# Front of a fused attention, expert and mixing kernel: second buffers for raw queries and keys, one block sum on VectorE, smaller constant load

## Chip, cores, metric

One Trainium2 chip, one core of it. The metric is device time in microseconds (us) for one execution; the time before is the median of 3 runs, 707.57 us (707.03 to 708.71).

## What is computed

Three stages in one launch, all in float32 at the interface. Only the first is touched by the change; the others follow it.

```python
# attention, B=2, H=8, S=768, D=64; nb = 24 blocks of 32 positions
k_sum = k.reshape(B, H, nb, block, D).max(axis=3)
v_sum = v.reshape(B, H, nb, block, D).mean(axis=3)
scores_l = scale * q @ k.T                  # kept where |i - j| < 16, else -1e9
scores_s = scale * q @ k_sum.T + log(block)
a = softmax(concat([scores_l, scores_s]))
x = a @ concat([v, v_sum])                  # (B, S, 512)
# experts: 8, one per token; argmax of x @ w_gate, held over from the token
# before where sigmoid(x @ w_local) >= 0.5; p[e] * (relu(x @ w1[e]) @ w2[e])
# mixing: u = x + real(fft(fft(x, seq), feature)); layer norm;
# out = u + relu(un @ w_ch1) @ w_ch2
```

## The kernel before, in words

Everything is written by hand for the five instruction streams: PE (matmul and transposes), VectorE, ScalarE, POOL (GpSimd) and SP, which only issues transfers. Each stream is in program order and waits on semaphores; the order of the work is the order of the code.

The attention stage goes over 8 **pairs** of heads (`PAIRS`) and in each over 6 **tiles** of 128 queries (`ST`). Pairs 0 to 5 run in a loop of three steps, two pairs in each (`par` is 0 or 1), pairs 6 and 7 behind it.

Raw queries and keys of a pair come in as `q_raw` and `k_raw` (one buffer each before), 192 KB per head and tensor (`load_qk`, L338). PE transposes them in three pieces (`stage`, L1205, the transposes on L1207) into a PSUM bank, ScalarE copies each piece out into `kT` and `qT` (L576, L580, L583). POOL lays `kT` out as windows (`k_win`, L464 to L469); VectorE takes the maxima over blocks of 32 keys (`block_max`, L793), and POOL copies them beside the windows (L476, L477). Pieces for pair i+1 are transposed in tiles 0 to 2 of pair i.

A tile goes: PE scores for both heads (L1234, 184 columns: 160 local and 24 block scores), VectorE adds the mask and takes the row maximum (`mask_scores`, L804), ScalarE the exponential with the row sums (L603), PE transposes the probabilities (L1243), VectorE copies them to SBUF (`probs_out`, L813), PE multiplies with the values (L1254 to L1256), VectorE normalises (L834). Sums are guarded and inverted for two tiles at once (L821, L827). Masks run two tiles ahead. The mask lies in the constants `cst` once for each head of a pair, since the second head has its 184 columns in another order.

The block means of the values: SP loads them with 32 positions of a block side by side (`load_blocks`, L358), 8 KB for each of 24 partitions and head, into `blocks`. The first pair's are summed by one VectorE instruction (L909), all others by POOL in five halving additions (`block_sums`, L489 and L493). The second pair's sum (`block_sums(1, 1, True)`) stands behind POOL's first key windows. ScalarE writes the means into the value tiles (`block_mean_rows`, L592) at the end of tile 5 of the pair before; for the first pair VectorE does it (L915). Both signal `vmean_ok`, which the pair's first value product waits for.

SP issues in this order: identity, keys, queries, the other constants, first blocks, first values (eight transfers, `load_v`, L345), second blocks, three tables of the gate; then, for each pair, keys and queries of the next pair as soon as PE has transposed this one's, blocks of the pair after next, values of the next pair.

In front, VectorE clears `qT`, `probs`, two columns of `x_all` and the edges of `kT` (L782, L783), signals `cleared`, and sends twelve increments to semaphores (L787). POOL clears `blocks`, `vA`, `vB` and `zero_row` (L453 to L456).

After attention come the gate (L1268 transposes, L1276 products; its first product waits for `tables_in`), the routing, the experts and the mixing.

## Time and profile before

| | |
|---|---|
| median of 3 runs | 707.57 us |
| the profiled execution, its own time | 704.34 us |
| its span, first to last instruction | 702.5 us |
| attention stage, by the timeline | about 0 to 110 us |
| PE busy over the span | 617.6 us (88%) |
| VectorE (DVE) busy | 359.5 us (51%) |
| ScalarE (ACT) busy | 259.5 us (37%) |
| POOL busy | 108.6 us (15%) |

Busy times are sums over one engine and overlap with the others. A row of a timeline gives the start in us from the span's start, the duration of the group, engine, source line and operation, what is written and read, how many instructions were merged (x4), and in brackets how long the engine was idle before and what released it. A windows row gives for one stretch the busy us (and instruction count) of PE, PE's weight loads, DVE, ACT and POOL, then the granted clock of TensorE, the busy share of the transfer engines and GB/s. In the names `arena`, `mid` and `small` are large SBUF tensors that hold many tiles (keys, queries, values and probabilities in `arena`, blocks and the row of zeros in `mid`), `bank` is PSUM, and `SPq` is SP's queue.

### The profile page before, as it was taken

To read this page: it belongs to the slowest core of one execution; us is meant where nothing else is said; L and a number is where in the kernel's file an instruction comes from. 1 tells how busy PE (TensorE), PEld (TensorE's weight loads), DVE (VectorE), ACT (ScalarE), POOL (GpSimd) and SP (SyncE) were. 2 spreads that over 40 slices of the span, in tenths; PEclk is the share of its full clock that TensorE was granted. 3 is DMA by queue.
4 is the path that set the end of the run, shared out by engine and by line. 5 is a ranking of instruction groups with operands and counts; after the bars stand their busy time and mean duration, and the time that the engine had idled before them with its cause. 6 is when DMAs were issued, how large, how long until landed. Compare 5 with 4: busy or idle time off the path is not lost.

```text
span 702.5 us, 11006 instructions
## 1 busy us (share of the span) xinstructions
PE 617.6 (88%) x3254; PEld 525.5 (75%) x3255; DVE 359.5 (51%) x893; ACT 259.5 (37%) x576; POOL 108.6 (15%) x132
## 2 busy tenths in 40 slices
PE   4799999411799899999889989999999999999994
PEld 3799999301578678878664468899899899989993
DVE  5788874743424252553326298444544454454442
ACT  3588874102313231441101133444344434434430
POOL 5657540033000010100100002002000040000001
PEclk9999999755889999999999999999999999999998
DMA  7766645046812381124141431000100010000001
GB/s 170 164 140 154 144 141 204 0 146 235 311 43 61 119 276 30 30 60 149 45 156 39 179 121 61 1 1 0 46 1 1 0 45 0 0 33 12 0 0 45
DMA packets 58874, 59.07 MB, mean 84 GB/s; under 512 B 43552, under 2 KB 43680, under 8 KB 57824
## 3 DMA queue, kind: packets, MB, share of 16 engines
q1 hardware_dynamic: 53056, 41.62, 19.7%
q0 software_dynamic: 3776, 13.44, 4.9%
q10 hardware_dynamic: 2016, 3.70, 2.4%
q8 instruction: 13, 0.21, 0.1%
q14 instruction: 13, 0.11, 0.1%
HBM read 43.73 MB, written 15.01 MB: 84 GB/s over the span
## 4 chain that ended last, share of the span: by engine, by line
PE 68%; DVE 9%; issue 8%; ACT 5%; DMA 5%; POOL 2%; SPq 2%; DVEq 1%; ACTq 0%; POOLq 0%
PE bank L1480 18%; PE bank L1467 18%; PE bank L1385 9%; PE bank L1357 7%; PE bank L1234 3%; ACT arena L603 3%; DMA mid<-sorted_x 2%; DVE parts L967 2%; PE bank L1243 2%; POOL sorted_x L516 1%; PE bank L1410 1%; PE bank L1276 1%; PE bank L1423 1%; PE bank L1345 1%; PE bank L1254 1%
## 5 line engine op out<-in xcount | busy, mean ns | idle before, releaser
L967 DVE TENSOR_TENSOR parts<-arena,parts 128x512 fp32r<-128x512 f32 (+1 forms) x152 | 111.5, 773 | 99.3 <-ACT parts L729 78.9
L1467 PE MATMUL bank<-parts 128*128 128x384 f32 x768 | 147.8, 341 | 2.8 <-DVE parts L967 2.8
L1480 PE MATMUL bank<-parts 128*128 128x512 f32 x576 | 143.7, 394 | 0.2
L1467 PEld LDWEIGHTS bank<-parts 128*128 128x128 f32 x768 | 136.8, 190 | 8.6 <-DVE parts L967 4.5
L1480 PEld LDWEIGHTS bank<-parts 128*128 128x128 f32 x576 | 106.8, 188 | 20.9 <-DVE mid L1130 1.1
L1385 PE MATMUL bank<-parts 128*128 128x512 f32 x312 | 77.1, 404 | 5.9 <-DVE parts L967 5.3
L1357 PE MATMUL bank<-parts 128*128 128x512 f32 x312 | 76.3, 401 | 2.1 <-DVE parts L967 2.1
L1385 PEld LDWEIGHTS bank<-parts 128*128 128x128 f32 x312 | 59.5, 194 | 20.0 <-issue 4.7
L729 ACT ACTIVATE parts<-arena 128x512 fp32r<-128x512 f32 x64 | 40.4, 631 | 83.5 <-PE bank L1480 83.5
L1357 PEld LDWEIGHTS bank<-parts 128*128 128x128 f32 x312 | 59.1, 193 | 14.6 <-issue 2.8
L967 DVE TENSOR_TENSOR parts<-bank,parts 128x512 fp32r<-128x512 f32 (+1 forms) x56 | 35.1, 649 | 42.4 <-ACT parts L719 19.7
L753 ACT ACTIVATE parts<-bank 128x384 fp32r<-128x384 f32 x64 | 31.5, 491 | 56.7 <-PE bank L1467 56.7
L1168 DVE SCALAR_TENSOR_TENSOR parts<-bank,parts 128x384 fp32r<-128x384 f32 x64 | 35.6, 557 | 30.9 <-ACT parts L753 30.9
L603 ACT ACTIVATE arena<-arena,small 128x184 f32<-128x184 f32 x96 | 42.1, 440 | 10.3 <-DVE small L804 9.3
L1234 PE MATMUL bank<-arena 128*128 128x184 f32 x192 | 41.1, 340 | 1.3 <-ACT arena L583 1.3
L523 POOL DMA_INDIRECT folded_y<-mid,dest_i x13 | 12.5, 958 | 180.0 <-DVE dest_i L1025 180.0
L724 ACT ACTIVATE parts<-arena 128x512 fp32r<-128x512 f32 x64 | 39.5, 618 | 0.0
L1345 PE MATMUL bank<-cst,mid 128*128 128x128 f32 x56 | 10.0, 308 | 31.9 <-DMA mid<-sorted_x 31.8
L551 POOL DMA_INDIRECT out<-mid,rows_i x6 | 6.1, 1020 | 205.0 <-DVE mid L1130 204.4
L1024 DVE TENSOR_SCALAR mid<-bank,small 128x512 f32<-128x512 f32 x13 | 9.8, 751 | 52.5 <-PE bank L1385 52.5
L489 POOL TENSOR_TENSOR mid<-mid 128x1024 f32<-128x1024 f32 (+3 forms) x28 | 33.7, 1202 | 12.9 <-DMA mid<-in_v 9.2
L1234 PEld LDWEIGHTS bank<-arena 128*128 128x128 f32 x192 | 31.6, 202 | 3.1 <-ACT arena L583 1.7
(174 smaller groups left out, 732.1 us busy)
## 6 DMA issues: line engine op xcount, KB each, us to landing
arena<-in_moe_w SPq DMA_DIRECT2D x24, 512.0 KB, 5.0
sorted_x<-mid POOLq DMA_DIRECT2D x1, 5160.0 KB, 18.3
arena<-in_moe_w_ch SPq DMA_DIRECT2D x2, 2048.0 KB, 8.3
arena<-in_moe_w_ch SPq DMA_DIRECT2D x4, 1024.0 KB, 8.9
mid<-sorted_x ACTq DMA_DIRECT2D x14, 258.0 KB, 3.2
arena<-in_k SPq DMA_DIRECT2D x16, 192.0 KB, 2.7
arena<-in_q SPq DMA_DIRECT2D x16, 192.0 KB, 3.2
mid<-in_v SPq DMA_DIRECT2D x16, 192.0 KB
```

Source lines behind the costliest of these rows:

```text
L489: pool.tensor_tensor(blocks[:, par, 0:n], blocks[:, par, 0:n], blocks[:, par, n:2 * n], ALU.add).then_inc(halved, 1)
L603: last = act.activation(probs[:, t % 3, (2 * NSP - NS) * hh:(2 * NSP - NS) * hh + NS], masked[:, t % 3, hh, :], ACT.Exp, scale=-1.0, bias= ...
L724: act.activation(m1_hi[:, f % 2, :].rearrange("p (c n) -> p c n", c=DC), m1_raw[:, :, P * f:P * f + P], ACT.Copy).then_inc(m1h_ok, 1)
L729: act.activation(m2_hi[:, f % 2, :], m2_raw[:, f, :], ACT.Copy).then_inc(m2h_ok, 1)
L753: act.activation(g_hi[:, f % 2, :], bank[2 + f % 2][:, 0:GN], ACT.Relu).then_inc(ghi_ok, 1)
L967: return dve.tensor_tensor(out, whole, upper.bitcast(F32), ALU.subtract)
L1168: dve.scalar_tensor_tensor(g_lo[:, f % 2, :], bank[2 + f % 2][:, 0:GN], 0.0, g_hi[:, f % 2, :].bitcast(F32), ALU.max, ALU.subtract).then_i ...
L1234: last = pe.matmul(S_BANK[t % 3][:, NS * hh:NS * hh + NS], qT[:, par, hh, P * t:P * t + P], k_win[:, par, t, keys], start=True, stop=True)
L1357: last = pe.matmul(bank[1 + half][:, :], x[:, r], w[:, c, f], start=(c == 0 and x is xT_hi and w is w1_hi), stop=(c == DC - 1 and w is w1_lo))
L1385: last = pe.matmul(bank[5][:, :], x[:, c, :], w[:, c // 2, f], start=(c == 0 and x is hT_hi and w is w2_hi), stop=(c == FC - 1 and w is w2 ...
L1467: last = pe.matmul(bank[2 + f % 2][:, 0:GN], w[:, f % 2, r], x[:, par, c, :], start=(c == 0 and w is m1_hi and x is cT_hi), stop=(c == DC ...
L1480: last = pe.matmul(bank[4 + t][:, :], x[:, f % 2, r], w[:, f % 2, :], start=(f == 0 and x is g_hi and w is m2_hi), stop=(f == MC - 1 and w ...
```

## The change

`q_raw` and `k_raw` get a second buffer, with a semaphore for each (`k_in`, `q_in` become pairs), and SP loads them one pair further ahead. The second pair's blocks are summed by VectorE in one instruction, inside tile 4 of the first pair (a branch around it in the other loop steps). The mask is loaded for the first head alone, and VectorE copies it into `mask2` in the second head's order. The constants that only the routing needs, and the gate's tables, are loaded behind the last values, the former for 8 partitions. VectorE clears `blocks`, and `probs` after the signal `cleared`; POOL clears `zero_row` first and of `vA` only the rows that no load fills. PE starts with two matmuls of 512 columns on `zero_row`, of which nothing is used. In front SP issues values ahead of blocks.

```diff
-    for name, n in (("ident", P), ("mask", 3 * 2 * NS), ("base", NT), ...
+    for name, n in (("ident", P), ("mask", 3 * NS), ("base", NT), ("forced", NT), ("first", E), ("dest", NT),
+                    ("iota", 1), ("thr", NT), ("tri", E), ("slot", SLOTS + 1), ("ones", 1), ("odd", CW), ("expert", E), ("sum", P)):
...
+        late_consts = cols["iota"][0]
-        q_raw = a(ST * P).rearrange("p (t h d) -> p t h d", t=ST, h=2)
+        q_raw = a(2 * ST * P).rearrange("p (b t h d) -> p b t h d", b=2, t=ST, h=2)
...
@@ SP @@
-            load_qk(0)
-            sp.dma_start(cst[:, P:], consts[:, P:]).then_inc(consts_in, 16)
+            load_qk(0, 0)
+            sp.dma_start(cst[:, P:late_consts], consts[:, P:late_consts]).then_inc(consts_in, 16)
             sp.wait_ge(v_cleared, 2)
+            load_v(0, 0)
             sp.wait_ge(blocks_set, 1)
             load_blocks(0, 0)
-            load_v(0, 0)
+            load_qk(1, 1)
             load_blocks(1, 1)
-            sp.dma_start(wg[:, :, 0:E], ...).then_inc(tables_in, 16)
-            sp.dma_start(wg[:, :, E:E + 1], ...).then_inc(tables_in, 16)
-            sp.dma_start(rows_i[:, :], rows).then_inc(tables_in, 16)
             def next_pair(i, par, more=True):
-                sp.wait_ge(qk_ps, 3 * (i + 1))
-                load_qk(i + 1)
                 if more:
+                    sp.wait_ge(qk_ps, 3 * (i + 1))
+                    load_qk(i + 2, par)
                     sp.wait_ge(vsum_ok, i + 1)
                     load_blocks(i + 2, par)
...
             next_pair(PAIRS - 2, 0, False)
+            sp.dma_start(cst[0:E, late_consts:], consts[0:E, late_consts:]).then_inc(tables_in, 16)
+            sp.dma_start(wg[:, :, 0:E], ...).then_inc(tables_in, 16)
+            sp.dma_start(wg[:, :, E:E + 1], ...).then_inc(tables_in, 16)
+            sp.dma_start(rows_i[:, :], rows).then_inc(tables_in, 16)
@@ POOL @@
-            pool.memset(blocks, 0.0).then_inc(blocks_set, 1)
-            pool.memset(vA, 0.0).then_inc(v_cleared, 1)
+            pool.memset(zero_row, 0.0).then_inc(zero_set, 1)
+            pool.memset(vA[0:PRE, :, 0], 0.0).then_inc(v_cleared, 1)
             pool.memset(vB, 0.0).then_inc(v_cleared, 1)
-            pool.memset(zero_row, 0.0).then_inc(zero_set, 1)
...
-                if first:
-                    pool.wait_ge(vsum_ok, 1)
-                else:
-                    pool.wait_ge(vmean_ok, i - 1)
+                pool.wait_ge(vsum_ok, i)
+                pool.wait_ge(vmean_ok, i - 1)
...
-            block_sums(1, 1, True)
@@ VectorE @@
-            for tile in (qT, probs, xa[:, :, DM + 2:XW], kT[:, 0:PRE]):
-                dve.memset(tile, 0.0)
-            link(dve.memset(kT[:, PRE + S:KTW], 0.0))
+            dve.memset(kT[:, 0:PRE], 0.0)
+            dve.memset(kT[:, PRE + S:KTW], 0.0)
+            link(dve.memset(qT, 0.0))
             dve.sem_inc(cleared, 1)
+            dve.memset(blocks, 0.0).then_inc(blocks_set, 1)
+            dve.memset(xa[:, :, DM + 2:XW], 0.0)
+            dve.memset(probs, 0.0).then_inc(rest_cleared, 1)
+            dve.wait_ge(rest_cleared, 1)
             for signal, n in ((att_out, TWO), (masked_ok, THREE), ...
                 dve.sem_inc(signal, n)
...
-  ... in1=mask[:, var_, hh, :],
+  ... in1=(mask, mask2)[hh][:, var_, :],
...
+            def add_blocks(par):
+                dve.tensor_reduce(block_sum[:, par], blocks[:, par].rearrange("p (j d) -> p d j", d=D), axis=AX.X, op=ALU.add).then_inc(vsum_ok, 1)
...
                     if t == 2 and not last_pair:
                         block_max(i + 1, 1 - par)
+                    if t == 4 and par == 0 and not last_pair and not isinstance(i, int):
+                        with dve.If(i < 1):
+                            dve.wait_ge(blocks_in[1], 32)
+                            add_blocks(1)
                 normalise(i, par, ST - 1, out_at(ST - 1))
             block_max(0, 0)
             dve.wait_ge(consts_in, 16)
+            for to, n, at in ((0, NB, WK), (NB, WK - P, P), (NS - P, P, 0)):
+                last = dve.tensor_copy(mask2[:, :, to:to + n], mask[:, :, at:at + n])
+            link(last)
...
             for b in range(B):
                 choose(b)
+            dve.wait_ge(tables_in, 64)
@@ PE @@
+            def keep_warm(columns, times):
+                for _ in range(times):
+                    pe.matmul(bank[0][:, 0:columns], zero_row[:, 0:P], zero_row[:, 0:columns], start=True, stop=True)
+            pe.wait_ge(zero_set, 1)
+            keep_warm(512, 2)
             pe.wait_ge(ident_in, 16)
...
-                    pe.wait_ge(k_in, 32 * (i + 1))
+                    pe.wait_ge(k_in[par], 32 * ((i + 2) // 2))
...
-                    pe.wait_ge(tables_in, 48)
+                    pe.wait_ge(tables_in, 64)
```

How the order of instructions changes at three places. VectorE in front, before:

```order
L782 MEMSET arena 128x3072
L782 MEMSET arena 128x1152
L782 MEMSET x_all 128x12x2
L782 MEMSET arena 128x15
L783 MEMSET arena 128x17
L793 TENSOR_REDUCE arena<-arena 128x24
L904 COPY x_all<-cst 128x12
```

and after the change:

```order
L781 MEMSET arena 128x15
L782 MEMSET arena 128x17
L783 MEMSET arena 128x3072
L785 MEMSET mid 128x4096
L786 MEMSET x_all 128x12x2
L787 MEMSET arena 128x1152
L797 TENSOR_REDUCE arena<-arena 128x24
L914 COPY mask<-cst 128x3x24
L914 COPY mask<-cst 128x3x32
L914 COPY mask<-cst 128x3x128
L918 COPY x_all<-cst 128x12
```

`mid 128x4096` is `blocks`, `arena 128x3072` is `qT`, `arena 128x1152` is `probs`. Clearing of `blocks` and three mask copies have come in, the clearing of `kT` has moved to the front.

SP in front, from the load of the constants on, before:

```order
L361 DMA cst<-consts 128x1712
L358 DMA mid<-in_v 24x2048 x2
L347 DMA arena<-in_v 113x64
L349 DMA arena<-in_v 128x5x64
L350 DMA arena<-in_v 32x5x64
L352 DMA arena<-in_v 15x64
L347 DMA arena<-in_v 113x64
L349 DMA arena<-in_v 128x5x64
L350 DMA arena<-in_v 32x5x64
L352 DMA arena<-in_v 15x64
L358 DMA mid<-in_v 24x2048 x2
L367 DMA wg_sb<-in_moe_w_gate 128x4x8
```

and now:

```order
L363 DMA cst<-consts 128x596
L349 DMA arena<-in_v 113x64
L351 DMA arena<-in_v 128x5x64
L352 DMA arena<-in_v 32x5x64
L354 DMA arena<-in_v 15x64
L349 DMA arena<-in_v 113x64
L351 DMA arena<-in_v 128x5x64
L352 DMA arena<-in_v 32x5x64
L354 DMA arena<-in_v 15x64
L360 DMA mid<-in_v 24x2048 x2
L343 DMA arena<-in_k 128x6x64 x2
L343 DMA arena<-in_q 128x6x64 x2
```

The eight value transfers stand ahead of the first blocks (`mid<-in_v`), keys and queries of the second pair follow these, and the tables are gone from here.

VectorE at the end of tile 4 and the start of tile 5 in a loop's first pair, before:

```order
L833 REGISTER_ALU
L834 ISA
L834 TENSOR_TENSOR x_all<-bank,small 128x128
L821 TENSOR_SCALAR small<-small 128x4
L813 COPY arena<-bank 128x384
L826 REGISTER_ALU
L827 RECIPROCAL small<-small 128x4
```

and now:

```order
L837 REGISTER_ALU
L838 ISA
L838 TENSOR_TENSOR x_all<-bank,small 128x128
L906 COMPARE_AND_BRANCH
L881 TENSOR_REDUCE small<-mid 128x64
L906 UNCONDITIONAL_BRANCH
L825 TENSOR_SCALAR small<-small 128x4
L817 COPY arena<-bank 128x384
L830 REGISTER_ALU
L831 RECIPROCAL small<-small 128x4
```

Between the normalisation of tile 3 and the guard of the sums there now stand a branch and the block sum.

## Rows read from the trace of the kernel before

**Rows 1.** Windows table, one settled head pair; columns in the section above
```profile
37.60:49.10 11.50, 11.36 (x92) 10.94 (x91) 9.46 (x44) 9.48 (x33) 7.18 (x11) 1.00 0.62 146
```

**Rows 2.** Chain of waits, 0 to 130 us: start us, us, what
```profile
17.94 3.03 DMA arena<-in_k
21.01 1.12 PE bank L1207 x4
```

**Rows 3.** Timeline of VectorE, front: start us, us, instruction, idle before
```profile
1.43 2.62 DVE L782 MEMSET arena<- 128x3072 f32 x1 [1.31 <-PEq L1528]
...
8.78 0.95 DVE L793 TENSOR_REDUCE arena<-arena 128x24 f32<-128x768 f32 x1 [3.44 <-ACT arena L583]
12.12 0.18 DVE L904 COPY x_all<-cst 128x12 f32<-128x12 f32 x1 [2.39 <-DMA cst<-consts]
13.03 0.35 DVE L804 CUSTOM_DVE_ANT_0 arena<-bank,cst 128x184 f32<-128x184 f32 x1 [0.73 <-PE bank L1234]
...
14.79 0.08 DVE L804 DVE_READ_ACCUMULATOR2_ANT small<- 128x1 f32 x1
14.79 3.62 DVE L909 TENSOR_REDUCE small<-mid 128x64 f32<-128x2048 f32 x1
...
19.19 0.56 DVE L813 COPY arena<-bank 128x384 f32<-128x384 f32 x1
...
20.32 1.74 DVE L821 TENSOR_SCALAR small<-small 128x4 f32<-128x4 f32 x1
```

**Rows 4.** Line 787 on VectorE's sequencer: count, ns min/median/max, first and last start
```profile
L787 DVEq EVENT_SEMAPHORE  x12: 21/21/21, 5.5 to 6.5; - x12
```

**Rows 5.** Timeline of PE, front
```profile
4.72 1.08 PE L1207 MATMUL bank<-cst,arena 128*128 128x128 f32 x4 [4.72 <-DMA arena<-in_k]
...
11.20 2.82 PE L1234 MATMUL bank<-arena 128*128 128x184 f32 x8 [1.28 <-ACT arena L583]
```

**Rows 6.** Timeline of ScalarE, exponentials of tiles 2 and 4, pairs 0 and 1
```profile
22.66 0.44 ACT L603 ACTIVATE arena<-arena,small 128x184 f32<-128x184 f32 x1
...
28.11 0.45 ACT L603 ACTIVATE arena<-arena,small 128x184 f32<-128x184 f32 x1
...
35.43 0.44 ACT L603 ACTIVATE arena<-arena,small 128x184 f32<-128x184 f32 x1
...
39.61 0.45 ACT L603 ACTIVATE arena<-arena,small 128x184 f32<-128x184 f32 x1
```

**Rows 7.** Timeline of POOL, front
```profile
6.79 0.53 POOL L456 MEMSET mid<- 128x516 f32 x1
...
10.18 0.31 POOL L477 COPY arena<-arena 128x144 f32<-128x144 f32 x1
19.69 2.34 POOL L489 TENSOR_TENSOR mid<-mid 128x1024 f32<-128x1024 f32 x1 [9.20 <-DMA mid<-in_v]
```

**Rows 8.** Timeline of SP, transfer issues in front and of the last values
```profile
7.67 0.25 SPq L347 DMA_DIRECT2D arena<-in_v  x1
...
14.68 0.77 SPq L358 DMA_DIRECT2D mid<-in_v  x2
...
95.39 0.44 SPq L352 DMA_DIRECT2D arena<-in_v  x1
```

**Rows 9.** Line 1207 (transposes of keys and queries), 0 to 20 us: ns min/median/max
```profile
L1207 PE MATMUL bank<-cst,arena x12: 417/421/474, 4.7 to 9.5; 128*128 128x128 f32 x12
```

**Rows 10.** The same line, 37 to 100 us
```profile
L1207 PE MATMUL bank<-cst,arena x64: 272/273/289, 37.7 to 95.5; 128*128 128x128 f32 x64
```

**Rows 11.** Timelines of VectorE, ScalarE and PE, end of the first pair
```profile
31.46 0.29 DVE L834 TENSOR_TENSOR x_all<-bank,small 128x128 f32 x1
...
31.02 1.06 ACT L592 ACTIVATE arena<-small 32x384 f32<-32x384 f32 x2
...
33.34 0.50 PE L1243 MATMUL bank<-cst,arena 128*128 128x128 f32 x3
```

**Rows 12.** Timeline of PE, first product of the gate
```profile
103.49 0.95 PE L1276 MATMUL bank<-wg_sb,mid 128*128 128x9 f32 x8
```

More of the change, by code:

```diff
@@ L94, in shape_constants @@
         mask[:, v, :WK][(np.abs(i - j) < WINDOW) & (j >= 0) & (j < S)] = 0.0
-    second = np.concatenate([mask[:, :, WK:], mask[:, :, P:WK], mask[:, :, :P]], 2)
-    put("mask", -np.stack([mask, second], 2))
+    put("mask", -mask)
     token = P * np.arange(NT)[None, :] + np.arange(P)[:, None]
```

32 lines of the change are left out of this document (16 added, 16 removed).

## Prediction

> **What bounds the kernel now.** The change touches the attention stage and what stands in front of it, so I read the timeline of that stage engine by engine, after the table of windows and the chain of waits. First the regime. In a settled head pair of 11.5 us, PE is busy 11.36 us, VectorE 9.46, ScalarE 9.48 [rows 1]. PE binds there, with work back to back, and two buffers, a shorter constant load or a spare POOL move nothing in it. The exponentials of query tile 4 start at 28.11 us in the first pair and at 39.61 us in the second [rows 6]: 11.5 us again, so the settled rate holds from the end of the first pair, and what the change can win or lose lies before it or is a stall put into it. I use the tile-4 exponential of the first pair, 28.11 us, as the mark.
>
> Second, what fills the 28.11 us. A settled pair needs 4 tiles of 1.92 us (11.5 over 6) from tile 0 to tile 4, 7.7 us; from the first exponential at about 13.8 us (after the first mask at 13.03 [rows 3]) that would be 21.5, so some 6.6 us are lost. In them stand, in this order: VectorE's sum of the first pair's value blocks, 14.79 to 18.41 us, ahead of everything that tile 0 still needs [rows 3]; and PE's wait for the second pair's raw keys until 21.01 [rows 2], which ScalarE inherits, its third exponential starting at 22.66 [rows 6]. The keys' transfer itself took 3.0 us [rows 2]; it was issued only behind the values, the second pair's blocks (at 14.68 [rows 8]) and three tables. Third, PE is at its lower clock level (1.2 of 2.4 GHz) in front. The granted clock column reads 1.00 in the attention stage [rows 1] but the first transposes take a median of 421 ns, settled ones 273 [rows 9, 10].
>
> **The change, part by part.** *The front.* VectorE now clears kT and qT, then the 4096 columns of blocks, then probs, and only then sends its twelve semaphore increments. Its memset of 3072 columns took 2.62 us [rows 3], so 4096 cost 3.5 and probs' 1152 cost 1.0. 1.43 + 2.6 + 0.2 + 3.5 + 0.1 + 1.0 is 8.9 us. The increments ran from 5.5 to 6.5 [rows 4], so 1.1 us more, now behind the clearing: 10.0. The first key maximum, at 8.78 before behind ScalarE [rows 3], moves to 10.1 and is the new last wait: 0.95 for it, then POOL's two copies as before (end of the maximum 9.73 to end of the copies 10.49 [rows 7], 0.8) give the first scores at 11.9 against 11.20 [rows 5]. **Mask copies:** three copies of 72, 96 and 384 columns stand on VectorE right behind the maximum. No row has them; the nearest are the copy of 12 columns at 0.18 us (below: three of these, 0.5) and the PSUM copy of 384 at 0.56 (above, with 0.2 for each small one: 1.0) [rows 3]. I take 0.8. VectorE has the time, the first mask can't start before 13. But they run while POOL copies key maxima. The trace has such a meeting: the 4-column operation at 20.32 took 1.74 us and ended with POOL's 2.34 us addition [rows 3, 7]; I take 0.4 us for POOL's delay, bounds 0 and 0.8. First scores at 12.3.
>
> The Trainium skill, page "SBUF — State Buffer", section "Who interferes with whom", says that VectorE and GpSimd share one port pair and that whoever issues first blocks the other wholly. By that rule POOL would lose up to the whole 0.8 us and the sum would be 0.4 us worse; the trace's 1.74 us row agrees with it.
>
> **Constants:** the load shrinks from 1840 to 724 columns. VectorE's wait for it until 12.12 was followed by a wait for PE until 13.03 [rows 3], so nothing is won on the path. Its worth is for the queue: values are issued from 3.9 us, not from 7.67. Eight issues took 7.0 us before (7.67 to 14.68 [rows 8]), less with a thinner backlog, so the first blocks go out at about 10, and land at 14.2 (the second pair's took 4.2 us from the end of issue, 15.45, to POOL's start at 19.69 [rows 7, 8]). **Warming matmuls:** two of 128x512 on zeros, from about 1.3 us (POOL starts at 0.7, and its memset of zero_row, 0.53 us [rows 7], now goes first). The front has no matmul of 512 columns; eight records of 184 columns took 2.82 us [rows 5], 352 ns each, so four records of 512 cost 3.4 to 3.9 us. They end at about 5.0 us against keys ready at 4.72 [rows 5]. That 0.3 is covered by VectorE's new lateness. If the clock is up afterwards, first scores to second mask shrinks from 3.67 us (11.20 to 14.87 [rows 3, 5]) to about 2.4, else nothing. In my forecast it is up: PE then has worked nearly without a gap from 1.4 to 6.2 us, longer than ahead of any of its early waits before.
>
> With the clock up the masks are done at 14.7, blocks have landed at 14.2, and the sum of the first blocks starts at 14.7: **no gain over 14.79**. The clearing on VectorE has eaten it. Tile 0's copy comes at 19.1 and the third exponential, held by VectorE's masks and not by keys (issued at 10.8, landed by 15), at 20.4 against 22.66: copy and masks take the 1.2 us from 19.19 to beyond 20.32 as before [rows 3]. From there to tile 4 the second pair needs 4.2 us (35.43 to 39.61 [rows 6]); the first took 5.45, with PE at the lower level for half of it. Mark at 24.6: **3.5 us earlier**.
>
> *The second pair's sum.* It leaves POOL (where it ran from 19.69 unseen) for VectorE, behind the normalisation of tile 3 in the first pair. That ended at 31.75, 3.64 us behind the mark [rows 11]. The sum is the same instruction as the first, 3.62 us [rows 3]. Queued behind it on VectorE: tile 5's copy and the second pair's masks. ScalarE waits for it too: its two mean copies (1.06 us, from 31.02 [rows 11]) stand ahead of the second pair's first exponential and now start 7.4 us behind the mark, end at 8.5; the exponentials take 1.0, and PE transposes them at 9.6 where it did at 33.34, 5.2 behind the mark [rows 11]. **Cost 4.4 us**, nothing of it won back where PE is busy 11.36 of 11.5. Bounds: 2.0 (if the idle 2 us of VectorE and ScalarE per pair [rows 1] take part of it up) and 4.8 (a branch that takes 0.4).
>
> *Second buffer.* Keys and queries go out one pair earlier on the same queue, the same bytes per pair: nothing in settled pairs. *Tables.* Four small loads move behind the last values, issued by 95.8 [rows 8], so out at 98 and, at 3 to 4 us each, landed by 102; the first use is at 103.5 [rows 12]. Hidden by 1.5 us. SP's weight loads behind them wait for the routing anyway. POOL's third sum now waits for VectorE's second; it is due a pair later.
>
> **Sum:** -3.5 + 4.4 = +0.9, and +0.1 for three branches on VectorE: +1.0 us. The profiled execution took 704.34 us (span 702.5), so 705.3 by its own time. It stands 3.2 us under the median of 707.57, and I carry the difference over: **708.6 us**. Within 0.2% (1.4 us, about what a measurement can tell) that is no change.
>
> **The rivals.** *A, the sum hides (faster).* VectorE and ScalarE idle 2 us in every pair [rows 1], POOL's late addition no longer collides with tile 1's operation of 1.74 us [rows 3]. If this takes half of the 4.4 us, the cost is 2.0 and the result -3.5 + 2.0 = -1.5: 706.1. Against it: ScalarE's order puts the mean copies ahead of the next exponential, and PE has no slack. *B, cold front (slower).* The zero matmuls end before the keys' transposes and PE stays at the lower level, as it did from 4.72 us on with waits between its bursts [rows 5, 9]. Then the second mask is done at 12.3 + 3.67 = 16.0, the first sum starts there, the third exponential at 21.7, and tile 4 follows 4.8 us later, at 26.5: gain 1.6, result -1.6 + 4.4 = +2.8, 710.4. It decides from the point at which the second mask ends after 15.2 us. *C, the tables come late (slower).* If they land after 103.5 [rows 12] the gate's first product waits; with values still in the queue I put that at 1 us, 709.6. *D, the port.* POOL's 2.36 us addition starts with the end of VectorE's second sum; should it come first, VectorE's next 4-column operation waits as it did for 1.74 us [rows 3]: +1.7, 710.3. The same section of the Trainium skill would have this decided by which of the two issues first. *E, the change doesn't do what it says:* first blocks behind the values land at 16, not 14.2, and the start isn't any earlier: +1.8, 710.4.
>
> **How the numbers follow.** Forecast 0.45, A 0.18, B 0.20, C 0.05, D 0.05, E 0.07. The forecast's own range is 706.9 to 709.9 (POOL's delay 0 to 0.8, cost 3.6 to 4.8, landing of the blocks 0.8 either way); to hold 8 in 10 the whole range runs from 706.2 to 710.8. Faster by over 0.2% is nearly A: 0.16. Slower is B, D, E and a quarter of the forecast, less what falls short of 709.0: 0.38. Within: 0.46.
>
> **What would show it.** VectorE's first key maximum at 10.1 us; first mask between 13 and 14; first block sum at 14 to 15; no PE wait for keys at tile 0; the tile-4 exponential of the first pair at 24 to 25.5; one VectorE sum of 3.6 us at about 28 and ScalarE's mean copies directly behind it; settled pairs of 11.5 us after that, and all beyond 126 us shifted only. The prediction is wrong if the mark isn't earlier, if PE's pause at the end of the first pair is under 3 us, or if a settled pair changes its length.

## Result and profile after

The changed kernel takes **709.86 us** (median of 13 runs, 705.48 to 715.24) against 706.17 us for the kernel before (median of 13 runs too, the first three among them). The ratio of the two is **1.0061, 95% interval 1.004 to 1.0082**: slower by about 4 us (the ratio is estimated over the runs; the two medians alone give 1.0052). The forecast was 708.6 us, "no change" the likeliest verdict; the time fell inside the range, the move was larger than forecast and outside what I had called no change.

The profiled execution took 710.31 us (span 708.5), 6.0 more than before's 704.34. Both kernels spread more from run to run than the first three runs had shown, and the profiled execution of before lies 1.8 us under its median, so below I compare kernels by marks in the trace first and by medians second. Three marks on ScalarE's timeline carry it: the exponential of tile 4 in the first pair ("first mark"), the same in the second pair ("second mark"), and the last exponential of the attention stage (at 114.61 us before, so the stage is some us longer than the 110 given ahead). The marks scatter by some tenths: the change, e4 and e12 have the same front, and their first marks are at 27.16, 26.84 and 26.84.

| us | before | after | difference |
|---|---|---|---|
| VectorE's first sum starts | 14.79 | 16.93 | +2.1 |
| third exponential | 22.66 | 23.02 | +0.4 |
| first mark | 28.11 | 27.16 | -0.95 |
| second mark | 39.61 | 44.78 | +5.17 |
| third pair's | 51.22 | 56.42 | +5.20 |
| last exponential | 114.61 | 120.08 | +5.47 |
| span | 702.5 | 708.5 | +6.0 |

Nearly all of it lies between the first and the second mark: 17.6 us where a settled pair takes 11.5. VectorE's timeline of the changed kernel (columns as in [rows 3]):

```profile
1.49 2.62 DVE L783 MEMSET arena<- 128x3072 f32 x1 [0.59 <-issue]
5.14 3.47 DVE L785 MEMSET mid<- 128x4096 f32 x1 [1.03 <-issue]
...
8.83 1.02 DVE L787 MEMSET arena<- 128x1152 f32 x1 [0.19 <-issue]
11.09 0.95 DVE L797 TENSOR_REDUCE arena<-arena 128x24 f32<-128x768 f32 x1 [1.24 <-ACT arena L583]
11.96 0.65 DVE L914 COPY mask<-cst 128x72 f32<-128x72 f32 x3
...
14.95 0.35 DVE L808 CUSTOM_DVE_ANT_0 arena<-bank,cst 128x184 f32<-128x184 f32 x1 [2.02 <-PE bank L1255]
...
16.93 3.67 DVE L881 TENSOR_REDUCE small<-mid 128x64 f32<-128x2048 f32 x1
20.64 1.03 DVE L929 TENSOR_SCALAR arena<-small 32x384 f32<-32x384 f32 x2
...
30.62 3.60 DVE L881 TENSOR_REDUCE small<-mid 128x64 f32<-128x2048 f32 x1
```

Against [rows 3] and [rows 4]: the clearing of the blocks (3.47) begins only at 5.14, behind 1.03 us in which the row gives no cause. The first key maximum is at 11.09, not 8.78; the first mask at 14.95, not 13.03; the first sum at 16.93, not 14.79. The last row is the sum that came from POOL. What released the first sum stands in the chain of waits (start us, us, what):

```profile
11.24 0.36 SPq L360
...
11.64 5.27 DMA mid<-in_v
16.93 3.68 DVE small L881
```

The first blocks were issued at 11.24 and landed at 16.91; the masks were done at 16.79. So two waits end almost together there, and the sum started on the landing. PE's timeline:

```profile
1.51 3.75 PE L1220 MATMUL bank<-mid 128*128 128x512 f32 x4 [1.51 <-POOL mid L457]
5.05 1.06 PE L1228 MATMUL bank<-cst,arena 128*128 128x128 f32 x4
6.89 0.63 PE L1228 MATMUL bank<-cst,arena 128*128 128x128 f32 x4 [0.78 <-ACT arena L576]
...
13.15 2.79 PE L1255 MATMUL bank<-arena 128*128 128x184 f32 x8 [3.84 <-POOL arena L480]
...
34.81 0.79 PE L1275 MATMUL bank<-arena 128*128 128x128 f32 x2 [3.07 <-DVE arena L817]
...
36.37 0.90 PE L1264 MATMUL bank<-cst,arena 128*128 128x128 f32 x3
```

The warming matmuls end at 5.26. The four transposes behind them still take 1.06 us, the next four 0.63, but the first scores take 2.79, near the 2.82 of [rows 5]. There is no wait for keys any more, which stood at 21.01 in [rows 2]. At 34.81 PE comes out of a pause of 3.07 us. ScalarE's rows, which answer to [rows 6] and [rows 11]:

```profile
23.02 0.45 ACT L603 ACTIVATE arena<-arena,small 128x184 f32<-128x184 f32 x1 [2.60 <-DVE small L808]
...
27.16 0.45 ACT L603 ACTIVATE arena<-arena,small 128x184 f32<-128x184 f32 x1
...
34.26 1.06 ACT L592 ACTIVATE arena<-small 32x384 f32<-32x384 f32 x2 [4.42 <-DVE small L881]
...
44.78 0.45 ACT L603 ACTIVATE arena<-arena,small 128x184 f32<-128x184 f32 x1
```

The mean copies wait 4.42 us until VectorE's sum (L881) releases them at 34.26. Last the table of windows, cut where the clock changes:

```profile
6.60:10.00 3.40, 1.29 (x8) 0.84 (x8) 3.06 (x3) 1.82 (x6) 1.59 (x4) 1.00 0.32 74
10.00:20.20 10.20, 6.18 (x22) 5.66 (x23) 6.32 (x14) 2.86 (x10) 0.69 (x2) 0.50 0.88 183
20.20:33.90 13.70, 9.46 (x72) 8.62 (x70) 12.30 (x38) 6.21 (x22) 2.15 (x6) 1.00 0.76 160
33.90:40.70 6.80, 5.87 (x23) 5.61 (x24) 3.80 (x18) 4.20 (x15) 5.50 (x6) 0.50 0.54 129
40.70:52.20 11.50, 11.26 (x91) 10.84 (x91) 8.82 (x43) 8.83 (x30) 6.81 (x11) 1.00 0.52 128
```

The granted clock (the column behind POOL's) is 1.00 from 6.6 to 10.0, then 0.50 to 20.2, 1.00, and **0.50 again from 33.9 to 40.7**: the pause has dropped TensorE from 2.4 to 1.2 GHz for 6.8 us in which PE is busy 5.87. In the kernel before the clock was at 1.00 from 24.6 us to the end of the stage.

### The profile page after: what moved, and what is told of

The parts are those of the page before. It is cut to its first block, busy times and chain, and to the rows that moved or that the text cites. A ratio compares the mean times of both kernels' runs of the same rounds, so it can differ in the third digit from the quotient of the medians.

```text
span 708.5 us, 11015 instructions
## 1 busy us (share of the span) xinstructions
PE 623.8 (88%) x3258; PEld 528.4 (75%) x3259; DVE 364.7 (51%) x898; ACT 259.4 (37%) x576; POOL 98.8 (14%) x126
## 3 DMA queue, kind: packets, MB, share of 16 engines
HBM read 43.18 MB, written 15.01 MB: 82 GB/s over the span
## 4 chain that ended last, share of the span: by engine, by line
PE 69%; DVE 10%; issue 7%; ACT 5%; DMA 5%; POOL 2%; SPq 2%; DVEq 1%; ACTq 0%; POOLq 0%
PE bank L1502 18%; PE bank L1489 17%; PE bank L1407 10%; PE bank L1379 7%; PE bank L1255 3%; ACT arena L603 2%; DVE parts L982 2%; DMA mid<-sorted_x 2%; PE bank L1264 2%; PE bank L1432 1%; PE bank L1297 1%; POOL sorted_x L516 1%; PE bank L1445 1%; PE bank L1275 1%; PE bank L1367 1%
## 5 line engine op out<-in xcount | busy, mean ns | idle before, releaser
L1489 PE MATMUL bank<-parts 128*128 128x384 f32 x768 | 146.3, 338 | 2.8 <-DVE parts L982 2.8
L729 ACT ACTIVATE parts<-arena 128x512 fp32r<-128x512 f32 x64 | 40.4, 631 | 84.5 <-PE bank L1502 84.5
L1367 PEld LDWEIGHTS bank<-cst,mid 128*128 128x128 f32 x56 | 7.4, 152 | 33.7 <-DMA mid<-sorted_x 32.2
```

What stands on the lines that cost most here:

```text
L729: act.activation(m2_hi[:, f % 2, :], m2_raw[:, f, :], ACT.Copy).then_inc(m2h_ok, 1)
L1367: last = pe.transpose(bank[0][:, P * c:P * c + P], xs[:, P * c:P * c + P], ident)
L1489: last = pe.matmul(bank[2 + f % 2][:, 0:GN], w[:, f % 2, r], x[:, par, c, :], start=(c == 0 and w is m1_hi and x is cT_hi), stop=(c == DC ...
```

## Experiments

Twelve kernels ran, in four groups on four chips; each ratio is against runs of the kernel before on the same chip, and one profile was kept of each. Marks are read from ScalarE's, VectorE's and PE's timelines of each profiled run.

| | first sum | first mark | second mark | last exp. | median us | ratio (95%) |
|---|---|---|---|---|---|---|
| before | 14.79 | 28.11 | 39.61 | 114.61 | | |
| after | 16.93 | 27.16 | 44.78 | 120.08 | 709.86 | 1.0061 (1.0040 to 1.0082) |
| e1 sum on POOL | 16.71 | 27.18 | 39.46 | 114.76 | 704.88 | 0.9987 (0.9959 to 1.0015) |
| e2 clearing on POOL | 15.22 | 25.14 | 43.53 | 118.91 | 709.33 | 1.0056 (1.0035 to 1.0076) |
| e3 both on POOL | 15.41 | 25.32 | 38.98 | 114.29 | 705.90 | 1.0000 (0.9971 to 1.0030) |
| e4 pause filled | 16.71 | 26.84 | 42.40 | 117.66 | 707.24 | 1.0018 (0.9990 to 1.0046) |
| e5 before, sum on VectorE | 14.83 | 28.99 | 47.02 | 122.09 | 712.45 | 1.0100 (1.0076 to 1.0124) |
| e6 before, two buffers | 14.95 | 26.32 | 44.05 | 119.38 | 709.18 | 1.0060 (1.0029 to 1.0090) |
| e7 e3, blocks ahead of keys | 14.99 | 27.32 | 38.67 | 113.96 | 704.99 | 0.9979 (0.9955 to 1.0004) |
| e8 e7, more warming | 15.01 | 27.54 | 38.90 | 114.18 | 704.28 | 0.9984 (0.9955 to 1.0014) |
| e9 e8, blocks first | 12.78 | 26.51 | 38.58 | 113.87 | 704.75 | 0.9982 (0.9959 to 1.0006) |
| e10 after, no warming | 16.70 | 26.84 | 44.62 | 119.92 | 708.54 | 1.0035 (1.0011 to 1.0058) |
| e11 e8, POOL waits | 15.65 | 27.15 | 38.75 | 114.05 | 702.50 | 0.9956 (0.9932 to 0.9980) |
| e12 after, sum in halves | 16.71 | 26.84 | 44.43 | 119.82 | 709.86 | 1.0055 (1.0025 to 1.0084) |

**e1: the second pair's sum back on POOL.**

```diff
+            block_sums(1, 1, True)          # POOL, behind keys(0, 0)
-                    if t == 4 and par == 0 ...:    # VectorE
-                        with dve.If(i < 1): ... add_blocks(1)
```

> The changed kernel with one part undone: the second pair's blocks are again summed by POOL behind its first key windows. Theory (the sum on VectorE stops ScalarE and PE at the end of the first pair for 4.0 us, and the clock that falls in the pause costs 2.1 us more): the tile-4 exponential of the second pair comes 11.5 us after that of the first, at about 38.7 instead of 44.8, and the kernel is 1 us faster than before (0 to 2), 5 to 6 faster than the change. Rival (the sum fits into VectorE's idle time and the loss has another source, such as second buffers or the order of the transfers): the tile-4 exponential stays beyond 42 us and the kernel stays 2 us or more slower than before.

The second mark is at 39.46, from 44.78; the kernel is 5 us faster than the change (704.88 against 709.86, medians of two chips) and not to be told from before. So the sum's place is the loss. But the theory's "1 us faster than before" isn't there: from mark to mark it takes 12.3 us, not 11.5. PE's timeline says why:

```profile
29.61 0.89 PE L1254 MATMUL bank<-arena 128*128 128x184 f32 x4 [0.86 <-POOL arena L480]
```

PE waits 0.86 us for POOL's key copies, which now queue behind a sum that started when its blocks had landed, at 21.50. The lower clock lasted longer in the front of this run (to 22.7 us), but the stall was gone: no pause of PE over 1 us stood between the two marks, and the clock stayed up to the end of the stage.

**e2: clearing of the blocks back on POOL**, behind its other clearing, the sum left on VectorE.

```diff
-            dve.memset(blocks, 0.0).then_inc(blocks_set, 1)
+            pool.memset(blocks, 0.0).then_inc(blocks_set, 1)
```

> The changed kernel with the clearing of the value blocks back on POOL, behind its other clearing; the second pair's sum stays on VectorE. Theory: VectorE is done with clearing and increments some 4.5 us earlier, the first key maximum starts behind ScalarE at about 8.7 instead of 11.09, the first sum at 14.0 to 14.8 instead of 16.93, and the mark (tile-4 exponential of the first pair) 2 us earlier; the kernel is 2 us faster than the change, still 2 to 3 slower than before. Rival (the first sum waits for its transfer, which lands at 14 to 16): first sum at 16 or later, gain under 1 us.

The key maximum is at 8.62, the first sum at 15.22 (a little later than expected), the first mark at 25.14, 2.0 us earlier, as the theory had it. The second mark gains 1.25 only, and the median 0.5, where 2 were expected. The stall behind the first mark was there again (PE waited 3.06 us, until 32.78), with the clock down from 33.6 to 40.4 us. All of these 6.8 us lie behind the pause, where in the change it was 5.9 (34.81 to 40.7); that this took the missing 0.8 us is likely and not tested. VectorE waited 0.89 us for its first blocks here, so the front now hangs on them.

**e3: both of these.**

(`block_sums(1, 1, True)` on POOL and `pool.memset(blocks, 0.0)`, the two diffs above together.)

> Both undone: clearing of the blocks and the second pair's sum on POOL. What is left of the change are the second buffers, the smaller constants, the mask copies, the warming matmuls and the tables behind the values. Theory: the two effects add, mark at about 25, second pair's at 36.5 to 37 against 39.61 before, kernel 3 us faster than before (2 to 4). Rival (the keys' wait was worth nothing because VectorE's first sum bounds tile 0 anyway): mark later than 27 and no gain over before.

The first mark is at 25.32, as expected, 2.8 us ahead of before. The second is at 38.98, 0.6 ahead: 2.2 us have gone between them. POOL's and PE's timelines:

```profile
21.03 2.35 POOL L493 TENSOR_TENSOR mid<-mid 128x1024 f32<-128x1024 f32 x1 [10.14 <-DMA mid<-in_v]
```

```profile
29.13 0.89 PE L1254 MATMUL bank<-arena 128*128 128x184 f32 x4 [2.24 <-POOL arena L481]
```

POOL had stood idle for 10.14 us until the second pair's blocks landed, added from 21.03 to 26.87, and only then did the second pair's key windows; PE waited 2.24 us for them. The gain of the front is handed to the next wait. In the kernel before, that POOL sum began at 19.69 [rows 7] and was hidden because everything else was late too.

**e4: three more matmuls in PE's pause**, on the row of zeros, into a bank that is free there; they compute nothing that is used.

```diff
+                if par == 0 and not last_pair and not isinstance(i, int):
+                    with pe.If(i < 1):
+                        pe.wait_ge(qk_sb, 6)
+                        keep_warm(512, 3, Q_BANK)
                 values(i, par, ST - 1)
```

> The changed kernel with three more matmuls of 512 columns on the row of zeros, issued by PE in the pause at the end of the first pair only (a branch in the loop). They compute nothing that is used. Theory (after the pause PE works at the lower clock for 6.8 us, which costs 2.1 us): the clock stays at 1.00 from about 20 us to beyond 120, the second pair's tile-4 exponential comes at 42.5 to 43 instead of 44.8, the kernel is 1.5 to 2 us faster than the change. Rival (the pause alone is the cost and the clock is not): no difference, or 0.3 slower for the branches.

PE's timeline and the windows of that run:

```profile
31.27 2.79 PE L1220 MATMUL bank<-mid 128*128 128x512 f32 x6
34.53 0.49 PE L1275 MATMUL bank<-arena 128*128 128x128 f32 x2 [0.47 <-DVE arena L817]
```

```profile
31.40:35.50 4.10, 3.54 (x13) 1.62 (x12) 3.88 (x9) 1.49 (x4) 1.29 (x1) 1.00 0.84 191
35.50:41.00 5.50, 4.91 (x40) 4.87 (x41) 3.66 (x16) 4.63 (x20) 4.79 (x8) 1.00 0.40 99
```

The clock stays at 1.00, the second mark comes at 42.40. From mark to mark: 15.56 us against 17.62 in the change and 11.5 settled. That splits the loss: **4.06 us for the stall itself, 2.06 for the clock** that it drops. The median moved by 2.6 us, the intervals overlap a little. Each part rests on one trace; the change, e10 and e12 took 17.62, 17.78 and 17.59 us from mark to mark, so take both as good to 0.2.

**e5: the sum on VectorE, alone, in the kernel before.**

```diff
-            block_sums(1, 1, True)
+                    if t == 4 and par == 0 ...:
+                        with dve.If(i < 1):
+                            dve.wait_ge(blocks_in[1], 32)
+                            dve.tensor_reduce(block_sum[:, 1], blocks[:, 1]..., op=ALU.add).then_inc(vsum_ok, 1)
```

> The kernel before with one part of the change alone: the second pair's blocks summed by VectorE in tile 4 of the first pair, as in the change. Theory (this part is a stall of 4 us, and more where the clock falls in it): the mark stays at 28.1 (less up to 0.5, since POOL no longer holds VectorE's 4-column operation for 1.74 us), the second pair's tile-4 exponential moves from 39.6 to 43.6 (45.5 with the clock down), and the kernel is 4 to 6 us slower than before. Rival (the stall arises only together with the faster front): under 2 us slower.

One per cent slower, 6.7 us: more than the whole change costs. PE's timeline:

```profile
36.78 0.80 PE L1255 MATMUL bank<-arena 128*128 128x128 f32 x2 [3.02 <-DVE arena L810]
```

The same pause, 3.02 us, and 18.0 us from mark to mark, with the clock at 0.50 from 36.4 to 43.2. The first mark was 0.9 later than before (the clock rose at 26.2 there and at 24.6 in the kernel before); the 0.5 that I expected from POOL's absence doesn't show. The rival is out.

**e6: two buffers for keys and queries, alone, in the kernel before.**

```diff
             load_v(0, 0)
+            load_qk(1, 1)
             load_blocks(1, 1)
```

> The kernel before with another part alone: two buffers for raw queries and keys, the second pair's loaded right behind the first values and ahead of the second blocks; all sums, clearing, constants and tables as before. Theory A (the keys' wait was worth 2 us, but POOL's sum of the second pair then starts later, at 21 to 22, and its key copies hold the scores of the second pair): third exponential at 20.5 to 21.5 instead of 22.66, the mark at 25.5 to 26.5, but the second pair's mark only at 38.8 to 39.5 against 39.61, kernel within 1 us of before. Theory B (nothing else is late): the second pair's mark at 37 to 38, kernel 2 us faster.

The third exponential is at 21.12 and the first mark at 26.32, as theory A had it. The rest I had too small by far: the second mark is at 44.05, the kernel 0.6% slower. POOL's and PE's timelines:

```profile
24.24 2.36 POOL L491 TENSOR_TENSOR mid<-mid 128x1024 f32<-128x1024 f32 x1 [13.57 <-DMA mid<-in_v]
```

```profile
32.35 1.59 PE L1236 MATMUL bank<-arena 128*128 128x184 f32 x4 [4.46 <-POOL arena L479]
```

The second pair's blocks land at 24.24 behind 768 KB of keys and queries (19.69 in [rows 7]), POOL adds until 30, and PE waits 4.46 us for the key windows, and the clock is at 0.50 from 29.4 to 36.2 us. So second buffers with the blocks behind the keys are a loss (e7 turns the order round). The change's sum on VectorE takes that wait away and puts another in its place.

**e7: e3 with the second pair's blocks issued ahead of its keys**, and POOL's halving additions no longer waiting for VectorE's sum.

```diff
-            load_qk(1, 1)
             load_blocks(1, 1)
+            load_qk(1, 1)
```

> A version meant to beat both: as the run with both parts on POOL, but SP issues the second pair's blocks ahead of its keys, and POOL does the four halving additions without waiting for VectorE's sum (only its last addition, which signals, waits). Theory (in that run PE's 2.24 us wait for POOL's key copies is POOL's sum, which started only at 21.03 when its blocks landed): the sum starts at 15 to 17 and ends by 22, the wait is gone, the mark stays at 25.3 to 26 and the second pair's comes 11.5 us later, at 37 to 37.5 instead of 38.98; kernel 2 to 3 us faster than before. Rival (the keys now land too late, or VectorE's small operations wait for POOL's additions): mark at 27 or later and no gain.

The wait for POOL is gone and the marks are 11.35 us apart. But the first mark fell back to 27.32: the rival's second half. VectorE's timeline:

```profile
14.99 3.60 DVE L884 TENSOR_REDUCE small<-mid 128x64 f32<-128x2048 f32 x1 [0.95 <-DMA mid<-in_v]
18.63 3.19 DVE L928 TENSOR_SCALAR arena<-small 32x384 f32<-32x384 f32 x2
```

and POOL's:

```profile
17.81 2.35 POOL L491 TENSOR_TENSOR mid<-mid 128x1024 f32<-128x1024 f32 x1 [7.95 <-DMA mid<-in_v]
20.34 1.27 POOL L491 TENSOR_TENSOR mid<-mid 128x512 f32<-128x512 f32 x1 [0.18 <-POOL mid L491]
```

VectorE waited until 14.99 for its blocks, and its two writes of 384 columns into 32 partitions took **3.19 us** where they take 0.7 or 1.0 in the runs above. They lie beside POOL's additions to 20.16 and to 21.61. The first half of the rival holds as well: PE waited 2.41 us for the second keys, until 18.60.

**e8: e7 with five more warming matmuls of 128 columns** between the first pair's pieces; they compute nothing that is used.

```diff
             for piece in range(3):
                 stage(0, 0, piece)
+                keep_warm(128, (1, 2, 2)[piece])
```

> The version before this one with five more matmuls of 128 columns on the row of zeros, one behind the first and two behind each of the other pieces of the first pair's transposes, which fill PE's waits there. They compute nothing that is used. Theory (two warming matmuls raised the clock in the run of the change from 6.6 to 10.0 us only, so that the first scores still took 2.79 us): the clock stays up, the first scores take 1.6 us, first sum 1 us earlier than without, and the kernel 1 us faster. Rival (the first sum is bound by the landing of its blocks at 14 to 15 us): the first scores are faster, the first sum isn't, no difference in the kernel.

```profile
10.83 1.49 PE L1254 MATMUL bank<-arena 128*128 128x184 f32 x8 [0.95 <-ACT arena L587]
```

The clock stays up from 6.0 to 16.3 and the first scores take 1.49 us instead of 2.79. The first sum is at 15.01 all the same, bound by its blocks (it waited 1.85 us for them). PE then waited 3.83 us for the second keys, and the clock fell at 16.3. The rival is right, and nothing is won.

**e9: e8 with the transfers in another order**: first blocks, second pair's keys, queries and blocks, then the first values.

```diff
-            sp.wait_ge(v_cleared, 2)
-            load_v(0, 0)
             sp.wait_ge(blocks_set, 1)
             load_blocks(0, 0)
-            load_blocks(1, 1)
             load_qk(1, 1)
+            load_blocks(1, 1)
+            sp.wait_ge(v_cleared, 2)
+            load_v(0, 0)
```

> The version with more warming, with another order of the front: POOL clears the blocks right behind the row of zeros, and SP issues first blocks, second pair's keys and queries, second pair's blocks, and only then the first values (behind the clearing of the value tiles). Theory (in the two runs before, VectorE's first sum waited for its blocks until 15.0, PE for the second keys until 18.7, and VectorE's two small operations behind the sum took 3.19 instead of 0.71 us while POOL added; all three follow from the order of the transfers): first sum at 12.6 to 13.2, no PE wait for keys, POOL's additions from 13 to 19, the mark at 23 to 24.5 and the second pair's at 34.5 to 36.5 against 39.61 before; kernel 3 to 4 us faster than before. Rival (the transfer engines are the bound of the front, so the values now come too late): PE waits for values until 19 to 21 at the first product, mark at 26 or later, kernel within 1 us of the run before.

The first sum starts at 12.78 without a wait, and there the theory ends. VectorE and PE:

```profile
16.52 3.37 DVE L928 TENSOR_SCALAR arena<-small 32x384 f32<-32x384 f32 x2
```

```profile
20.80 0.80 PE L1274 MATMUL bank<-arena 128*128 128x128 f32 x2 [4.33 <-DMA arena<-in_v]
```

Again 3.37 us for the two writes, beside POOL's addition, and now PE waits 4.33 us until the values have landed. Whichever transfer goes last is what the front waits for: the rival, with the mark at 26.51. The second mark, 38.58, is the earliest of all runs, by 0.1 us over e7.

**e10: the change without its warming matmuls.**

```diff
-            pe.wait_ge(zero_set, 1)
-            keep_warm(512, 2)
```

> The changed kernel without its two warming matmuls. Theory (they end before the transposes and the clock is down again at 10 us, so they are worth 0.4 us at two pieces that nothing waits for): first mask within 0.3 us of 14.95, the mark within 0.5 of 27.16 apart from where the clock rises, kernel within 1 us of the change. Rival (they bring the clock's rise at 20.2 forward): clock rises later than 22 and the mark is 1 us or more later.

First mask at 14.94, first mark at 26.84, clock up at 20.2 as with them. The two matmuls are worth nothing on the path; the pieces of transposes behind them take 1.09 and 1.11 us without them and 0.63 and 0.66 with them, and nobody waits for that.

**e11: e8 with POOL's first addition behind VectorE's two writes.**

```diff
-                if not first:
-                    pool.wait_ge(vmean_ok, i - 1)
+                pool.wait_ge(vmean_ok, 1 if first else i - 1)
```

> The version with more warming, but POOL starts its additions for the second pair only when VectorE has written the first pair's means. Theory (POOL's additions lock VectorE's two small writes out, 3.19 and 3.37 us instead of 0.71): the two writes take 0.7 to 1.1 us, third exponential at 20.5 to 21, the mark at 24.7 to 25.5 against 27.54; POOL's sum then runs from 19.5 to 25.3 and PE waits 1 to 2 us for the second pair's key copies, second pair's mark at 38 to 38.5, kernel equal to the run without this wait or up to 1 us faster. Rival (the two writes were slow by something else, such as transfers into the same tile): they stay over 2 us.

```profile
15.65 3.57 DVE L881 TENSOR_REDUCE small<-mid 128x64 f32<-128x2048 f32 x1 [2.38 <-DMA mid<-in_v]
19.26 0.71 DVE L925 TENSOR_SCALAR arena<-small 32x384 f32<-32x384 f32 x2
...
21.14 1.48 DVE L825 TENSOR_SCALAR small<-small 128x4 f32<-128x4 f32 x1
```

```profile
20.24 2.35 POOL L490 TENSOR_TENSOR mid<-mid 128x1024 f32<-128x1024 f32 x1 [9.56 <-DVE arena L925]
```

```profile
19.40 1.11 PE L1224 MATMUL bank<-cst,arena 128*128 128x128 f32 x4 [4.34 <-DMA arena<-in_k]
```

The two writes take 0.71 us: POOL was what held them. The next meeting follows, the 4-column operation at 21.14 takes 1.48 beside POOL's addition. The third exponential, at 21.34, is 2 us earlier than in e8; then the mark loses all but 0.4 of it, because the second keys came at 19.40 and the clock was down from 17.6 to 24.5. By the marks this kernel is 0.9 us ahead of before at the second pair and 0.6 at the end of the stage. Its median of 702.50 (0.9956, interval 0.9932 to 0.998) is the only one of the study clearly below before, but it is one of twelve, and its interval overlaps those of e7, e8 and e9, whose marks are nearly the same. I can place 0.6 of its 2.8 us.

**e12: the change with the sum cut in two**, 16 positions in tile 3, the rest and a 64-column addition in tile 4.

```diff
-                    if t == 4 and par == 0 ...: ... add_blocks(1)
+                    if t in (3, 4) and par == 0 ...:
+                            dve.tensor_reduce(halves[:, h], blocks[:, 1, n * h:n * h + n]..., op=ALU.add).then_inc(half_ok, 1)
+                            if t == 4:
+                                dve.wait_ge(half_ok, 2)
+                                dve.tensor_tensor(block_sum[:, 1], halves[:, 0], halves[:, 1], ALU.add).then_inc(vsum_ok, 1)
```

> The changed kernel with the second pair's sum cut in two on VectorE: 16 of 32 positions in tile 3 of the first pair, the rest and one addition of 64 columns in tile 4. Theory (nothing takes the stall up, since PE has no slack): from the mark to the second pair's mark at least 15.5 us, as 15.56 in the run with the filled pause, since what VectorE does is the same; kernel within 1 us of the change. Rival (masks run two tiles ahead, so that a stall of 1.8 us is partly absorbed twice): from tile 2's exponential of the first pair to tile 4's of the second 2 us less than in the change (19.7 less 2.4 for the clock), PE pauses under 1 us each, the clock stays up, kernel 3 us faster than the change.

```profile
28.63 1.93 DVE L910 TENSOR_REDUCE small<-mid 128x64 f32<-128x1024 f32 x1
...
31.67 1.86 DVE L910 TENSOR_REDUCE small<-mid 128x64 f32<-128x1024 f32 x1
```

```profile
31.07 0.49 PE L1280 MATMUL bank<-arena 128*128 128x128 f32 x2 [0.27 <-DVE arena L818]
...
34.41 0.80 PE L1280 MATMUL bank<-arena 128*128 128x128 f32 x2 [2.46 <-DVE arena L818]
```

PE's pauses are 0.27 and 2.46 us, 2.7 together instead of 3.07, and the marks 17.59 us apart instead of 17.62. The pause of 2.46 us was followed by the lower clock too (0.50 from 33.6 to 40.4 us). Masks running two tiles ahead take up a part of the first half, but ScalarE still stands before the mean copies until the whole sum is there (4.31 us, until 33.83). No difference from the change in the kernel: the theory holds, the rival doesn't.

## Why the prediction was right or wrong

**Right, and shown.** *The second pair's sum is a stall at the end of the first pair.* Forecast 4.4 us with bounds 2.0 and 4.8; e4 measured 4.06 with the clock held up. The path that the forecast took, from the sum over ScalarE's mean copies to the next exponential and on to PE, is the chain of waits of e4. In the change itself the chain goes from the sum over VectorE's copy of tile 5 to PE at 34.81, and from there PE at the lower clock sets the pace. ScalarE's wait (4.42 us) stands beside it. No run moves the mean copies, so what their place alone costs is not shown. *Rival A*, VectorE's idle time taking up half: out, by e1, e5 and e12. *Settled pairs* kept their 11.5 us. *The keys' wait* went, and from the third exponential to the first mark it took 4.14 us where 4.2 was forecast. *The smaller constants*: no wait for them stands on the path of either kernel; no run takes them out alone. *The gate's tables* were there in time: no wait stands before the first product, so rival C is out. *Rival D*: VectorE's 4-column operation behind its sum went first (0.16 us, as in a settled pair), POOL's addition started at 34.49 behind it.

**Wrong in size: the front.** The step put the first scores at 12.3, the masks at 14.7, the landing of the first blocks at 14.2 and the first sum at 14.7, with the mark 3.5 us earlier. Measured: scores at 13.15, masks done at 16.79, blocks landed at 16.91, first sum at 16.93, mark 0.95 earlier.

On the side of the masks: 0.85 us until the first scores, from the 1.03 us in front of the memset of the blocks, which no row of before could show; 1.2 us from there to the second mask, since the scores ran at the lower clock, 2.79 us where the upper gives 1.49 (e8). The step "In my forecast it is up" failed here: the clock rose at 6.6 us and was down again at 10.0.

On the side of the blocks: the eight value loads took 7.0 us to issue once more (4.17 to 11.20) where the forecast had less, the blocks went out at 11.24 instead of 10, and landed 4.9 us after the end of their issue (12.00) instead of 4.2. That is *rival E*: it had them land at 16. It cost only 0.1 to 0.2 us, because the masks were late as well (the first sums of e4, e10 and e12 start right behind their masks, at 16.70 or 16.71). Either side alone would have held the sum near where it was, and e8 shows it: with the clock up the scores were fast and the sum waited for its blocks.

Behind the sum, the two small writes took 1.03 us instead of 0.71. A copy of key windows by POOL starts at 20.59 in the change, and where it meets the writes (the change, e4, e10, e12) they take 0.93 to 1.03 us; in before, e1, e2 and e3 it doesn't, and they take 0.71. POOL's delay by the mask copies, for which I took 0.4 us, was small: its first copy starts 0.17 us behind the maximum and takes 0.43 instead of 0.31. e2 puts the price of the clearing on VectorE at 2.0 us of the first mark (1.7 against the 26.84 of e4, e10 and e12).

**Missing: the clock after the stall.** The forecast counted PE's pause as time lost once. It also dropped TensorE to 1.2 GHz from 33.9 to 40.7 us, and e4 measured 2.06 us for that. No step of the prediction asked what a pause of 3 us does to the clock, although the trace of before has PE at the lower level after its own early waits. At the second mark -0.95 + 4.06 + 2.06 is the measured +5.17 (it adds up by construction, since e4 splits the same 6.12 us in two), against a forecast of +0.9.

**Rival B** named the cold front and gave +2.8; its condition, a second mask ending after 15.2 us, was met (16.79), and its mark of 26.5 is nearer to the 27.16 than the forecast's 24.6. It was right about the scores at the lower clock, though the level was up from 6.6 to 10.0 us in between; it missed the same mechanism one pair later. That the time stayed inside 706.2 to 710.8 is luck. The terms came out 4.3 us worse at the second mark (front 2.55 and clock 2.06 worse, stall 0.34 better). But the medians moved by 3.7 us only, where the profiled executions lie 6.0 apart, and the kernel before had a median of 706.17 in 13 runs and not 707.57; 3.7 us on top of 707.57 would have been 711.3.

**What stays open.** The 1.03 us before the clearing of the blocks. They stand in all five runs with that memset on VectorE (the change, e1, e4, e10, e12); in e2, e3 and e9, where the small memset of `x_all` follows behind the same wait, it starts after 0.18 us. So they go with that instruction, and why is open. Why e11 gains 2.8 us in the median and 0.6 at the end of the stage. And small gains in the medians: e2 ends the stage 1.2 us ahead of the change and e3 0.5 us ahead of e1, and their medians are 0.5 lower and 1.0 higher: from the routing on, the clock falls and rises at moments that differ from run to run, and a microsecond in front can't be followed through.

## What to carry to other kernels

A sum that is hidden on a slow engine (POOL took 5.8 us for it in e3) isn't made cheaper by being 2.2 us shorter on an engine whose order others wait on: put it where nothing queues behind it. And ask of a PE pause not only how long it is but what it does to the clock: behind pauses of 3.07 us (the change) and 2.46 us (e12) the clock was down for 6.8 us, behind one of 2.24 us (e3) it stayed up. Where the front of a kernel is filled with transfers, a second buffer lets one transfer go ahead of another, so ask which one becomes the last and who waits for that (here POOL's sum, 4.46 us of PE). And in a chain of short waits, measure the next wait before removing the first: of the 2.8 us that e3 won in the first pair, the second pair kept 0.6.

## What the runs showed of the hardware

In the change a pause of 3.07 us on PE went with 6.8 us at a granted clock of 0.50 (from 33.9 us, the pause ending at 34.81), and filling it with 2.79 us of matmuls on zeros kept the clock at 1.00. PE lost the upper level in the front too, at 10.0 us in the change, between its last transposes (8.65) and the first scores (13.15). The Trainium skill ("TensorE: Matmul & The Clock Gate", Part 1) has the throttled clock as the default that activity lifts; both rows agree.

POOL's additions lengthen VectorE's small operations on SBUF: 3.19, 3.40 and 3.37 us (e7, e8, e9) instead of 0.71 for two writes of 384 columns; 1.48 us (e11), 1.58 (e1) and 1.74 [rows 3] instead of 0.16 for one of 4 columns, each of these three ending within 0.03 us of POOL's addition. The reductions (3.57 to 3.70 us) and the masks (0.35) beside them don't change. With POOL held back in e11 the writes took 0.71, so POOL's addition was what held them. The Trainium skill's rule ("SBUF — State Buffer", "Who interferes with whom": one shared port pair, held for the whole instruction) fits these rows; that it is a port that POOL holds no run tests.

The same issue can take SP three times as long. In the change the two query loads of the second pair took 3.54 us to issue, 1.13 for the first pair's, while the transfer engines were busy for 0.88 of the time (10.0 to 20.2 us). The second pair's blocks, which now stand behind them, went out at 16.64 instead of 14.68 [rows 8]:

```profile
2.22 1.13 SPq L343 DMA_DIRECT2D arena<-in_q  x2
...
13.06 3.54 SPq L343 DMA_DIRECT2D arena<-in_q  x2
16.64 0.98 SPq L360 DMA_DIRECT2D mid<-in_v  x2
```

Twelve semaphore increments in a row took 1.1 us on VectorE's sequencer [rows 4]. Before, a wait for ScalarE covered them; in the change they stand between the last memset and the first key maximum.
